# Two layers of experts with Strassen-like products on one core: the order of one sum on VectorE, and two products' tokens split by GpSimd

## The chip, the cores and the metric
The kernel runs on one core of a Trainium2 chip. The metric is the device time of one execution in microseconds; the time of a version is the median of its runs. The profile is of one further execution.

## What is computed
Attention with 4 sink keys and a window of 128, then a mixture of four experts with given weights, then a gated layer `h * cos(h)`. All values are fp32.

```python
x = attention(q, k, v)                  # 2 x 768 tokens, 8 heads of 64: x is 1536 x 512
p = domain_probs / (domain_probs.sum(-1, keepdims=True) + 1e-09)
for e in range(4):                      # w1[e]: 512 x 1024, w2[e]: 1024 x 512
    out += p[:, e:e + 1] * (np.maximum(x @ w1[e], 0.0) @ w2[e])
h = out @ w_in                          # 512 x 2048
result = (h * np.cos(h)) @ w_out        # 2048 x 512
```

## The kernel before
**Precision.** Each fp32 operand is split into a high part (rounded to the type fp32r) and a low part (operand minus high part, also fp32r). A product is then three matmuls: high by high, low by high, high by low (L1278, L1280, L1282 in the first layers; L1306, L1308, L1310 in the second). Making a split is a cast and a subtraction.

**Stages.** After the attention (to about 100 us) the work runs in 24 stages in four blocks. A block is one half of the tokens (768) in one layer pair: stages 0 to 7 and 8 to 15 are the experts for the first and the second half of the tokens, stages 16 to 19 and 20 to 23 the gated layers for the same halves. `FIRST = (0, 8, 16, 20)` holds the first stage of each. A stage takes 512 columns of the first weight and 512 rows of the second, and has two halves, a = 2s and b = 2s + 1.

**First layer of a half.** It is done with seven products of half matrices in place of eight (numbers 1 to 7; 6 matmuls of 128x384 each). The inputs of some are sums of blocks of x (`t_sum`) and of w1 (`w1_sum`), made by GpSimd. The products accumulate along a chain of PSUM banks: 1, then 6, 5 and 3 on top of it in `chain_bank`; 2 in `two_bank`; 7 and then 4 in `side_bank`. Between two of the chain ScalarE copies the bank out: `keep_1` (L694, after product 1), `keep_2` (L701, after 6), `keep_3` (L708, after 5). VectorE makes the four quarters of the result: `add_11` (L994), `add_22` (L1002, from product 7 and `keep_3`), `add_21` (L1010). Product 4 is written on top of `side_bank`, which `add_22` reads, so it waits for `add_22` of its half (L1271).

**Then** each quarter goes through the relu and is split: in an expert stage `relu_hi` on ScalarE (L725), `relu_lo` on VectorE (L1014). In a gated stage it is `whole` (L733), `fraction` (L1022), `fold` (L739), `cosine` (L744), `gate` (L1029), `gated_hi` (L752), `gated_lo` (L1035). `down` (L1306 to L1310, 36 matmuls for each half, 6 for each of six token tiles) is the second layer. VectorE adds the result of each of the six tiles to `acc` with `keep_down` (L1044 to L1050).

**Queues.** Each engine executes its instructions in the order in which they stand in the program; that order is written out by hand. TensorE in a stage: products a1, a2, a6, a7, a5, b1, a3, a4, b6, b2, b5, b7, b3, b4, then `down` of half a and of half b. Names in the rows: `scores` are PSUM banks 0 to 3, `bank` the banks 4 to 7, so product 4 of half b writes a `bank` and product 3 of half b a `scores`. The weights are split in each stage: `first_hi` on ScalarE (L669) and `first_lo` on GpSimd (L555) for w1, in three parts for each half; `second_hi` (L679) and `second_lo` (L562) for w2. GpSimd makes the sums of the next stage's w1 (`sum_weights`, L541 to L550) ahead of its `first_lo`.

**Opening of a block.** At the end of a block (`closes(s)`) the tokens of the next are split for all seven products: `tokens_hi` on ScalarE (L687), `tokens_lo` on VectorE (L952), in the order of `PRODUCTS = (1, 2, 6, 7, 5, 3, 4)`; each is 128x768 elements. At the end of stage 19, VectorE runs products 1 and 2's `tokens_lo`, then alternates the six `keep_down` with the other five, and then begins stage 20 with `add_11(a)`. ScalarE's stage 20 begins with `keep_1(a)`, then `whole` (which waits for `add_11(a)`), then `keep_2(a)`, on which product 5 of half a waits.

Of the kernel before, what the change touches and what calls it, by code (L numbers as in the profile page):

```python
# [5 lines left out]
ALU = mybir.AluOpType  # L6
ACT = mybir.ActivationFunctionType
AX_X = mybir.AxisListType.X
F32 = mybir.dt.float32
# [21 lines left out]
PRODUCTS = (1, 2, 6, 7, 5, 3, 4)  # L31


def program(nc, q, k, v, domain_probs, w1, w2, w_in, w_out, out, routing):
# [8 lines left out]
    TPB = S // P  # L43
# [20 lines left out]
    FIRST = (0, NE, 2 * NE, 2 * NE + NM)  # L64
    NS = 2 * NE + 2 * NM
    DOWN_ORDER = (3, 4, 5, 0, 1, 2)
    TURN_AT = {0: FIRST[1], 1: FIRST[2]}
    SUM_AT = {FIRST[1] - 2: 1, FIRST[2] - 2: 2, FIRST[3] - 1: 3}
    GATED = ((0, 11), (0, 22), (0, 12), (0, 21), (1, 22), (1, 12), (1, 11), (1, 21))

    def block_of(s):
        return sum(s >= first for first in FIRST) - 1
# [26 lines left out]
    with ExitStack() as ctx:  # L99
# [3 lines left out]
        def sem(name):  # L103
            return ctx.enter_context(nc.semaphore(name))

        x_hi = sb("x_hi", [P, 7, 2, HALF], F32R)
# [111 lines left out]
        x_summed = sem("x_summed")  # L218
        x_hi_ready = sem("x_hi_ready")
        x_lo_ready = sem("x_lo_ready")  # L220
        product_done = {n: sem(f"product{n}_done") for n in PRODUCTS}
        kept1 = sem("kept1")
        kept2 = sem("kept2")
# [58 lines left out]
        def x_block(block, n):  # L282

            g = block % 2
            low, high = slice(0, HALF), slice(HALF, S)
            if n in (1, 2):
                return x_t[:, g, 2 * (n - 1):2 * n, low]
            if n == 3:
                return x_t[:, g, 2:4, high]
            if n == 5:  # L290
                return x_t[:, g, 0:2, high]
            return t_sum[:, {6: 0, 7: 1, 4: 2}[n]]

        def w1_part(half, part):

# [132 lines left out]
        def _(pool):  # L428
# [102 lines left out]
            def sum_weights(s, n):  # L531

                low, high = slice(0, FS // 2), slice(FS // 2, FS)
                a11, a12 = w1_raw[:, 0:2, low], w1_raw[:, 2:4, low]
                a21, a22 = w1_raw[:, 0:2, high], w1_raw[:, 2:4, high]
                s2, s3, s4 = (w1_sum[:, i] for i in range(3))
                if n == 0:
                    pool.wait_ge(w1_landed, 16 * (s + 1))
                    if s >= 1:
                        pool.wait_ge(w1_lo_ready, 6 * s)  # L540
                    nc.gpsimd.tensor_tensor(s3, a11, a21, ALU.subtract).then_inc(w1_summed, 1)  # L541
                elif n == 1:
                    pool.wait_ge(w1_summed, 4 * s + 1)
                    nc.gpsimd.tensor_tensor(a21, a21, a22, ALU.add).then_inc(w1_summed, 1)
                elif n == 2:
                    pool.wait_ge(w1_summed, 4 * s + 2)
                    nc.gpsimd.tensor_tensor(s2, a21, a11, ALU.subtract).then_inc(w1_summed, 1)
                else:
                    pool.wait_ge(w1_summed, 4 * s + 3)
                    nc.gpsimd.tensor_tensor(s4, a12, s2, ALU.subtract).then_inc(w1_summed, 1)  # L550
# [14 lines left out]
            def sum_tokens(b, n):  # L565
# [20 lines left out]
                else:  # L586
                    pool.wait_ge(x_summed, 4 * b + 3)
                    nc.gpsimd.tensor_tensor(t4, b21, t2, ALU.subtract).then_inc(x_summed, 1)

            for i in range(ROUNDS + 3):  # L590
                if i % 2 == 0 and 0 <= (i - 2) // 2 < T and later((i - 2) // 2):
                    gather_sinks((i - 2) // 2)
                if 0 <= i - TURN_LAG < ND:
                    part_weights(i - TURN_LAG)
                if i == 0:
                    sink_keys(0)
                    sink_keys(1)
                    spread_values(0)
                elif i % 2 == 1 and (i + 3) // 2 < T:
                    sink_keys((i + 3) // 2)  # L600
                if i in (3, 2 * TPB + 2):
                    lower_values(i // TPB // 2)
                if i == 9:
                    spread_values(1)
                if 5 <= i < 9:
                    sum_weights(0, i - 5)
                if 10 <= i < 16:
                    first_lo(*divmod(i - 10, 3))
                if i % 2 == 0 and 0 <= (i - 6) // 2 < T:
                    normalise((i - 6) // 2)  # L610
                if 17 <= i < 21:
                    sum_tokens(0, i - 17)

            for s in range(NS):
                second_lo(s, 0)
                second_lo(s, 1)
                if s in SUM_AT:
                    for n in range(4):
                        sum_tokens(SUM_AT[s], n)
                if s + 1 < NS:  # L620
                    for n in range(4):
                        sum_weights(s + 1, n)
                    for h in (2 * s + 2, 2 * s + 3):
                        for part in range(3):
                            first_lo(h, part)

        @block.scalar
        def _(act):
# [52 lines left out]
            def tokens_hi(b, i):  # L681

                n = PRODUCTS[i]
                act.wait_ge(x_summed, 4 * (b + 1))
                if b >= 1:
                    act.wait_ge(product_done[n], 2 * FIRST[b])
                nc.scalar.activation(x_hi[:, n - 1], x_block(b, n), ACT.Copy).then_inc(x_hi_ready, 1)  # L687
# [184 lines left out]
        def _(dve):  # L872
# [75 lines left out]

            def tokens_lo(b, i):
                n = PRODUCTS[i]  # L950
                dve.wait_ge(x_hi_ready, 7 * b + i + 1)
                nc.vector.tensor_tensor(x_lo[:, n - 1], x_block(b, n), x_hi[:, n - 1].bitcast(F32), ALU.subtract)\  # L952
                    .then_inc(x_lo_ready, 1)

# [34 lines left out]
            def add_11(h):  # L989

                dve.wait_ge(product_done[2], h + 1)
                dve.wait_ge(kept1, h + 1)
                c = two_bank[h % 2][:, 0:HALF]
                nc.vector.tensor_tensor(c, c, kept[:, h % 2], ALU.add).then_inc(c11_ready, 1)  # L994
# [67 lines left out]
            for s in range(NS):  # L1062
                a, b = 2 * s, 2 * s + 1
                n = 8 * (s - FIRST[2])
                add_11(a)
                if is_gated(s):
                    fraction(n)
                    gate(n)
                    add_22(a)
                    gated_lo(n)  # L1070
                    fraction(n + 1)
                    fraction(n + 2)
                    add_21(a)
                    add_11(b)
                    gate(n + 1)
                    gate(n + 2)
                    fraction(n + 3)
                    add_22(b)
                    gated_lo(n + 1)
                    gated_lo(n + 2)  # L1080
                    fraction(n + 4)
                    gate(n + 3)
                    fraction(n + 5)
                    add_21(b)
                    gated_lo(n + 3)
                    gate(n + 4)
                    fraction(n + 6)
                    gated_lo(n + 4)
                    gate(n + 5)
                    fraction(n + 7)  # L1090
                    gated_lo(n + 5)
                    gate(n + 6)
                    gate(n + 7)
                    gated_lo(n + 6)
                    gated_lo(n + 7)
                else:
                    relu_lo(a, 11)
                    add_22(a)
                    relu_lo(a, 22)
                    relu_lo(a, 12)  # L1100
                    add_21(a)
                    relu_lo(a, 21)
                    add_11(b)
                    relu_lo(b, 11)
                    add_22(b)
                    relu_lo(b, 22)
                    relu_lo(b, 12)
                    add_21(b)
                    relu_lo(b, 21)
                if closes(s):  # L1110
                    for i in range(2 if is_gated(s) else 5):
                        tokens_lo(block_of(s) + 1, i)
                for k in range(TPB):
                    keep_down(s, k)
                    if closes(s) and is_gated(s) and k < 5:
                        tokens_lo(block_of(s) + 1, k + 2)
                    elif closes(s) and k < 2:
                        tokens_lo(block_of(s) + 1, k + 5)
                for i in range(len(turned_tiles(s))):
                    keep_turned(s, i)  # L1120

        @block.tensor
        def _(pe):
# [118 lines left out]
            def product(h, n):  # L1242

                s, i = divmod(h, 2)
                if opens(s) and i == 0:
                    pe.wait_ge(x_lo_ready, 7 * block_of(s) + PRODUCTS.index(n) + 1)
                pe.wait_ge(w1_lo_ready, 3 * h + (1 if n in (1, 2) else 2 if n in (7, 6, 3) else 3))
                if n == 1:
                    target, first = chain_bank[i], True
# [166 lines left out]
```

## Time and profile before
| | us |
|---|---|
| median of the runs | 863.89 |
| lowest and highest of the runs | 863.51, 864.95 |
| the profiled execution, its own time | 860.06 |
| its span, first to last instruction | 858.3 |
| TensorE matmul busy | 842.5 (98% of the span) |
| VectorE busy | 461.1 (54%) |
| ScalarE busy | 458.7 (53%) |
| GpSimd busy | 541.1 (63%) |
| mean granted clock of TensorE | 0.996 |

The engines' names in rows are PE (TensorE matmul), PEld (its weight loads), DVE (VectorE), ACT (ScalarE), POOL (GpSimd), SP (SyncE). A row of the timeline has the start in us from the span's start, the duration in us, engine, line, operation, output and inputs, shapes, the number of instructions merged into it, and in brackets the idle time before it with what ended it. Matmuls are pipelined: the durations of neighbours overlap, so the step from one start to the next is what one costs.

### The profile page before, as it was taken

The page shows a single profiled execution, that of the slowest core. Times are in us where ns is not written, and L with a number is a line of the kernel's source. Part 1 is how long each engine was busy: PE and PEld are TensorE (multiplying, and loading weights), DVE is VectorE, ACT ScalarE, POOL GpSimd, SP SyncE. Part 2 cuts the span into 40 slices and gives each one's busy share as a digit, 9 for nine tenths or more (in the row PEclk, how much of TensorE's full clock was granted, in tenths as well). Part 3 has the DMA queues.
Part 4 walks back from the last instruction along what each step waited for, and adds up shares of the span by engine and source line. Part 5 has one row for each costly group of instructions (what it writes and reads, how often), then busy time and mean ns, then how long its engine had stood idle before and what let it go on. Part 6 is the DMA issues. An engine that isn't in the chain of part 4 may idle for free.

```text
span 858.3 us, 13943 instructions
## 1 busy us (share of the span) xinstructions
PE 842.5 (98%) x4756; PEld 751.0 (87%) x4756; DVE 461.1 (54%) x952; ACT 458.7 (53%) x984; POOL 541.1 (63%) x408
## 2 busy tenths in 40 slices
PE   8899899999999999999999999999999999899998
PEld 6788789989988988988988998998898998898997
DVE  6678633433433427533433433348757759747756
ACT  6587734334334336423423423526867869767864
POOL 3699776556466775675475475867385396584450
PEclk9999999999999999999999999999999999999999
DMA  9794331211311220321131121120220230530201
GB/s 168 175 204 114 98 99 50 99 50 50 99 52 48 98 72 27 99 99 35 65 99 39 60 99 50 50 99 26 73 99 19 81 99 1 173 99 3 96 0 74
DMA packets 73156, 67.31 MB, mean 78 GB/s; under 512 B 40608, under 2 KB 46848, under 8 KB 73088
## 3 DMA queue, kind: packets, MB, share of 16 engines
q1 hardware_dynamic: 73088, 66.42, 26.0%
q8 instruction: 40, 0.66, 0.3%
q14 instruction: 28, 0.23, 0.1%
HBM read 62.96 MB, written 3.19 MB: 77 GB/s over the span
## 4 chain that ended last, share of the span: by engine, by line
PE 90%; issue 3%; DVE 2%; POOL 1%; ACT 1%; DMA 1%; SPq 1%; ACTq 0%; POOLq 0%
PE scores L1278 11%; PE scores L1282 10%; PE scores L1280 10%; PE scores L1308 10%; PE scores L1310 10%; PE scores L1306 10%; PE bank L1308 5%; PE bank L1310 5%; PE bank L1306 5%; PE bank L1278 3%; PE bank L1282 3%; PE bank L1280 3%; PE bank L1224 2%; PE scores L1187 1%; DVE x_lo L952 1%
## 5 line engine op out<-in xcount | busy, mean ns | idle before, releaser
L555 POOL TENSOR_TENSOR w_lo<-w_raw,w_hi 128x512 fp32r<-128x512 f32 x96 | 128.6, 1349 | 184.3 <-ACT w_hi L669 184.3
L1278 PE MATMUL scores<-x_hi,w_hi 128*128 128x384 f32 x528 | 178.6, 338 | 4.0 <-ACT kept L701 2.6
L1282 PE MATMUL scores<-x_hi,w_lo 128*128 128x384 f32 x528 | 177.3, 336 | 0.0
L1280 PE MATMUL scores<-x_lo,w_hi 128*128 128x384 f32 x528 | 177.3, 336 | 0.0
L562 POOL TENSOR_TENSOR w_lo<-w_raw,w_hi 128x1024 fp32r<-128x1024 f32 x48 | 116.8, 2444 | 65.6 <-ACT w_hi L679 65.6
L679 ACT ACTIVATE w_hi<-w_raw 128x1024 fp32r<-128x1024 f32 x48 | 50.7, 1059 | 189.7 <-PE scores L1310 189.7
L1308 PE MATMUL scores<-w_lo,h_hi 128*128 128x512 f32 x384 | 149.7, 390 | 0.0
L1310 PE MATMUL scores<-w_hi,h_lo 128*128 128x512 f32 x384 | 149.7, 390 | 0.0
L1306 PE MATMUL scores<-w_hi,h_hi 128*128 128x512 f32 x384 | 149.4, 389 | 0.0
L1278 PEld LDWEIGHTS scores<-x_hi,w_hi 128*128 128x128 f32 x528 | 99.6, 189 | 6.4 <-issue 5.6
L1050 DVE SCALAR_TENSOR_TENSOR acc<-scores,probs,acc 128x512 f32<-128x512 f32 x56 | 41.8, 749 | 116.3 <-PE scores L1310 116.3
L1280 PEld LDWEIGHTS scores<-x_lo,w_hi 128*128 128x128 f32 x528 | 99.7, 189 | 0.6
L1282 PEld LDWEIGHTS scores<-x_hi,w_lo 128*128 128x128 f32 x528 | 99.7, 189 | 0.0
L555 POOL TENSOR_TENSOR w_lo<-w_sum,w_hi 128x768 fp32r<-128x768 f32 x48 | 92.5, 1927 | 3.1 <-ACT w_hi L669 3.1
L1310 PEld LDWEIGHTS scores<-w_hi,h_lo 128*128 128x128 f32 x384 | 72.1, 188 | 15.0
L1306 PEld LDWEIGHTS scores<-w_hi,h_hi 128*128 128x128 f32 x384 | 72.1, 188 | 14.2
L1308 PEld LDWEIGHTS scores<-w_lo,h_hi 128*128 128x128 f32 x384 | 72.1, 188 | 14.2
L1308 PE MATMUL bank<-w_lo,h_hi 128*128 128x512 f32 x192 | 74.8, 390 | 0.0
L1310 PE MATMUL bank<-w_hi,h_lo 128*128 128x512 f32 x192 | 74.8, 389 | 0.0
L1306 PE MATMUL bank<-w_hi,h_hi 128*128 128x512 f32 x192 | 74.7, 389 | 0.0
L1014 DVE SCALAR_TENSOR_TENSOR h_lo<-bank,h_hi 128x384 fp32r<-128x384 f32 x64 | 35.7, 558 | 47.0 <-ACT h_hi L725 47.0
L1014 DVE SCALAR_TENSOR_TENSOR h_lo<-scores,h_hi 128x384 fp32r<-128x384 f32 x64 | 35.5, 555 | 47.3 <-ACT h_hi L725 45.8
(126 smaller groups left out, 1582.4 us busy)
## 6 DMA issues: line engine op xcount, KB each, us to landing
w_raw<-in_moe_w_dram SPq DMA_DIRECT2D x32, 1024.0 KB, 5.1
w_raw<-in_moe_w_in_dram SPq DMA_DIRECT2D x8, 1024.0 KB, 5.0
w_raw<-in_moe_w_out_dram SPq DMA_DIRECT2D x8, 1024.0 KB, 5.1
v_nat<-in_v_dram SPq DMA_DIRECT2D x12, 256.0 KB, 3.5
norm<-routing_dram SPq DMA_DIRECT2D x24, 128.0 KB, 3.2
out_dram<-acc SPq DMA_DIRECT2D x12, 256.0 KB, 4.2
k_nat<-in_k_dram SPq DMA_DIRECT2D x11, 256.0 KB, 4.8
q_nat<-in_q_dram SPq DMA_DIRECT2D x11, 256.0 KB, 5.2
```

Source lines behind the costliest of these rows:

```text
L555: nc.gpsimd.tensor_tensor(w1_slots(w1_lo, h % 2, part), w1_part(h % 2, part), w1_slots(w1_hi, h % 2, part).bitcast(F32), ALU.subtract)\
L562: nc.gpsimd.tensor_tensor(w2_lo[:, i::2], w2_raw[:, i::2], w2_hi[:, i::2].bitcast(F32), ALU.subtract)\
L679: nc.scalar.activation(w2_hi[:, i::2], w2_raw[:, i::2], ACT.Copy).then_inc(w2_hi_ready, 1)
L1014: nc.vector.scalar_tensor_tensor(h_part(h_lo, h % 2, c), c_source(h % 2, c), 0.0, h_part(h_hi, h % 2, c).bitcast(F32), ALU.max, ALU.subtract)\
L1050: kept_one = nc.vector.scalar_tensor_tensor(acc[:, n], down_bank[k][:], probs[:, n, e:e + 1], acc[:, n], ALU.mult, ALU.add)
L1224: last = nc.tensor.matmul(out_bank[r * D:(r + 1) * D, cols], v_nat[:, (t - 1 + part) % 3, head:head + D], weights_t[:, d % SLOTS, part, 2 ...
L1278: nc.tensor.matmul(target[:, 0:HALF], w1_hi[:, i, slot, d], x_hi[:, n - 1, d], start=first and d == 0, stop=False, skip_group_check=True)
L1280: nc.tensor.matmul(target[:, 0:HALF], w1_hi[:, i, slot, d], x_lo[:, n - 1, d], start=False, stop=False, skip_group_check=True)
L1282: last = nc.tensor.matmul(target[:, 0:HALF], w1_lo[:, i, slot, d], x_hi[:, n - 1, d], start=False, stop=d == 1, skip_group_check=True)
L1306: nc.tensor.matmul(down_bank[k][:], h_hi[:, i, f, toks], w2_hi[:, c], start=i == 0 and f == 0, stop=False, skip_group_check=True)
L1308: nc.tensor.matmul(down_bank[k][:], h_hi[:, i, f, toks], w2_lo[:, c], start=False, stop=False, skip_group_check=True)
L1310: last = nc.tensor.matmul(down_bank[k][:], h_lo[:, i, f, toks], w2_hi[:, c], start=False, stop=i == 1 and f == 1, skip_group_check=True)
```

## The change
1. **Expert stages, VectorE.** In half b, `add_22(b)` now stands ahead of `relu_lo(b, 11)` in place of behind it. The gated stages' order is not touched.
2. **Last block, GpSimd.** The splits of the tokens of products 1 and 2 of block 3 (the one that opens with stage 20) are made by GpSimd, cast and subtraction both, with semaphores of their own. They stand in its queue behind stage 20's `sum_weights` and ahead of its `first_lo`. ScalarE and VectorE leave them out, and the counts on which VectorE and TensorE wait are adapted.

```diff
+    SPLIT_BY_POOL = (1, 2)
...
+        def by_pool(block, n):
+            return block == 3 and n in SPLIT_BY_POOL
+
+        def splits_before(block, i):
+            return 7 * block + sum(not by_pool(block, n) for n in PRODUCTS[:i])
...
+            def split_tokens(b):
+                for m, n in enumerate(SPLIT_BY_POOL):
+                    pool.wait_ge(x2_ready, TPB * (b - 1))
+                    pool.wait_ge(product_done[n], 2 * FIRST[b])
+                    nc.gpsimd.tensor_copy(x_hi[:, n - 1], x_block(b, n)).then_inc(x_hi_ready_pool, 1)
+                    pool.wait_ge(x_hi_ready_pool, m + 1)
+                    nc.gpsimd.tensor_tensor(x_lo[:, n - 1], x_block(b, n), x_hi[:, n - 1].bitcast(F32), ALU.subtract)\
+                        .then_inc(x_lo_ready_pool, 1)
...
                     for n in range(4):
                         sum_weights(s + 1, n)
+                    if s + 1 == FIRST[3]:
+                        split_tokens(3)
                     for h in (2 * s + 2, 2 * s + 3):
...
             def tokens_hi(b, i):
                 n = PRODUCTS[i]
+                if by_pool(b, n):
+                    return
...
             def tokens_lo(b, i):
                 n = PRODUCTS[i]
-                dve.wait_ge(x_hi_ready, 7 * b + i + 1)
+                if by_pool(b, n):
+                    return
+                dve.wait_ge(x_hi_ready, splits_before(b, i) + 1)
...
                     add_11(b)
+                    add_22(b)
                     relu_lo(b, 11)
-                    add_22(b)
                     relu_lo(b, 22)
...
                 if opens(s) and i == 0:
-                    pe.wait_ge(x_lo_ready, 7 * block_of(s) + PRODUCTS.index(n) + 1)
+                    if by_pool(block_of(s), n):
+                        pe.wait_ge(x_lo_ready_pool, SPLIT_BY_POOL.index(n) + 1)
+                    else:
+                        pe.wait_ge(x_lo_ready, splits_before(block_of(s), PRODUCTS.index(n)) + 1)
```

## Rows read from the trace of the kernel before

**Rows 1.** The page, busy times: share of the span and instructions.
```profile
PE 842.5 (98%) x4756; PEld 751.0 (87%) x4756; DVE 461.1 (54%) x952; ACT 458.7 (53%) x984; POOL 541.1 (63%) x408
```

**Rows 2.** Waits of the weight loads: us in total, times, longest.
```profile
PEld bank L1278 <- issue: 5.2, 16, 0.3
```

**Rows 3.** Timeline of TensorE, stage 1: ends of products 7 and 3, start of 4.
```profile
139.87 0.33 PE L1282 MATMUL bank<-x_hi,w_lo 128*128 128x384 f32 x1
...
140.91 0.34 PE L1282 MATMUL scores<-x_hi,w_lo 128*128 128x384 f32 x1
141.29 0.41 PE L1278 MATMUL bank<-x_hi,w_hi 128*128 128x384 f32 x1
141.54 0.34 PE L1280 MATMUL bank<-x_lo,w_hi 128*128 128x384 f32 x1
```

**Rows 4.** Timeline of TensorE at the opening of stage 20.
```profile
730.61 0.34 PE L1282 MATMUL scores<-x_hi,w_lo 128*128 128x384 f32 x1
733.60 0.41 PE L1278 MATMUL scores<-x_hi,w_hi 128*128 128x384 f32 x1 [2.65 <-ACT kept L701]
```

**Rows 5.** Windows: length, busy PE, PEld, DVE, ACT, POOL, granted clock, DMA, GB/s.
```profile
86.20:89.60 3.40, 1.97 (x22) 1.47 (x22) 3.23 (x13) 3.40 (x13) 2.72 (x5) 1.00 0.27 68
...
734.70:738.10 3.40, 3.40 (x13) 3.40 (x12) 1.98 (x4) 2.03 (x5) 3.10 (x3) 0.51 0.33 67
```

**Rows 6.** Timeline of ScalarE, VectorE and weight loads at the same place.
```profile
139.20 0.49 ACT L708 ACTIVATE kept<-scores 128x384 f32<-128x384 f32 x1 [1.21 <-PE scores L1282]
...
140.11 0.56 DVE L1014 SCALAR_TENSOR_TENSOR h_lo<-bank,h_hi 128x384 fp32r<-128x384 f32 x1 [1.05 <-ACT h_hi L725]
140.58 0.56 DVE L1002 TENSOR_TENSOR bank<-bank,kept 128x384 f32<-128x384 f32 x1
...
141.26 0.19 PEld L1278 LDWEIGHTS bank<-x_hi,w_hi 128*128 128x128 f32 x1 [0.33 <-issue]
```

**Rows 7.** Timeline, gated stage 19: end of product 7, the sum, product 4.
```profile
707.98 0.33 PE L1282 MATMUL bank<-x_hi,w_lo 128*128 128x384 f32 x1
...
708.35 0.57 DVE L1002 TENSOR_TENSOR bank<-bank,kept 128x384 f32<-128x384 f32 x1
...
709.19 0.34 PE L1278 MATMUL bank<-x_hi,w_hi 128*128 128x384 f32 x1
```

**Rows 8.** Timeline of ScalarE, VectorE and TensorE, end of stage 19.
```profile
717.70 1.58 ACT L687 ACTIVATE x_hi<-x_t 128x768 fp32r<-128x768 f32 x2
...
718.58 1.91 DVE L952 TENSOR_TENSOR x_lo<-x_t,x_hi 128x768 fp32r<-128x768 f32 x2 [0.17 <-ACT x_hi L687]
...
719.57 0.39 PE L1310 MATMUL scores<-w_hi,h_lo 128*128 128x512 f32 x1
...
720.41 0.68 DVE L1046 TENSOR_TENSOR acc<-scores,acc 128x512 f32<-128x512 f32 x1
...
727.50 2.00 DVE L952 TENSOR_TENSOR x_lo<-x_t,x_hi 128x768 fp32r<-128x768 f32 x1
729.43 0.68 DVE L1046 TENSOR_TENSOR acc<-bank,acc 128x512 f32<-128x512 f32 x1
730.03 1.45 DVE L952 TENSOR_TENSOR x_lo<-t_sum,x_hi 128x768 fp32r<-128x768 f32 x1
...
732.00 0.55 DVE L994 TENSOR_TENSOR scores<-scores,kept 128x384 f32<-128x384 f32 x1
```

**Rows 9.** Timeline of GpSimd, end of stage 19.
```profile
717.51 1.29 POOL L555 TENSOR_TENSOR w_lo<-w_raw,w_hi 128x512 fp32r<-128x512 f32 x1 [5.50 <-ACT w_hi L669]
...
728.64 2.02 POOL L555 TENSOR_TENSOR w_lo<-w_raw,w_hi 128x512 fp32r<-128x512 f32 x1
```

**Rows 10.** Groups of GpSimd by shape: busy us, mean ns of one, idle before.
```profile
L480 POOL TENSOR_SCALAR_AFFINE_SELECT weights_t<-weights_t 128x512 f32<-128x512 f32 x20 | 13.5, 673 | 0.0
...
L585 POOL TENSOR_TENSOR t_sum<-x_t 128x768 f32<-128x768 f32 x4 | 7.4, 1845 | 0.2
...
L491 POOL CAST sink_w<-weights 128x64 fp32r<-128x64 f32 x10 | 3.1, 308 | 0.0
```

More of the change, by code:

```diff
@@ L220, in program @@
         x_lo_ready = sem("x_lo_ready")
+        x_hi_ready_pool = sem("x_hi_ready_pool")
+        x_lo_ready_pool = sem("x_lo_ready_pool")
         product_done = {n: sem(f"product{n}_done") for n in PRODUCTS}
```

## The prediction, made before the change was run
> **What bounds the kernel now.** I read the page's busy times first, then the waits, then the timeline engine by engine. The page gives TensorE 842.5 us of a span of 858.3 us [rows 1]. So the time is TensorE's own, plus the places where it stands still; a change on another engine counts only through such a place. The matmuls of the first layers (L1278, L1280, L1282) start 0.173 us apart when nothing holds them, those of the second (L1306 to L1310) 0.227 us. I went through all starts after 103 us and looked for larger steps. Three kinds matter here.
>
> First, one small step in each of the 16 expert stages, always ahead of product 4 of half b; the list of waits has it as 16 idle stretches of the weight load for `bank` that sum to 5.2 us [rows 2]. In one stage the start at 140.91 should be followed at 141.08 and 141.26; the profile has 141.29 and 141.54 [rows 3]. The second shows what is really lost, 0.285 us: 16 x 0.285 = 4.55 us.
>
> Second, one large stand at the opening of stage 20, the last block: last start 730.61, next 733.60 instead of 730.78, 2.82 us lost [rows 4].
>
> Third, behind this stand the granted clock is about half (0.51, the 1.2 GHz level) for 3.4 us [rows 5]; against 2.4 GHz that costs 3.4 x 0.49 = 1.65 us.
>
> **Part 1, the order on VectorE in an expert stage.** Nothing is added or removed: `add_22(b)` and `relu_lo(b, 11)` change places, 16 times. Before, ScalarE's copy of product 5 ends at 139.69 and TensorE's product 7 at 139.87 + 0.33 = 140.20 [rows 3, 6]. That is all `add_22(b)` needs, but `relu_lo(b, 11)`, started at 140.11, stands ahead of it in the queue, so it starts at 140.58 and ends at 141.14; the weight load follows 0.12 us later, at 141.26 [rows 6]. In the new order it starts 0.04 us behind product 7, at 140.24, ends at 140.80, and the load can go at 140.92. On time would be 140.91: the matmul comes on its beat. The gated stages already have that order, and show it: product 7 ends at 707.98 + 0.33 = 708.31, `add_22` starts at 708.35 and takes 0.57, and product 4 starts at 709.19, on the beat of 0.173 [rows 7]. So the whole step goes: **-4.55 us**. What it costs: `relu_lo(b, 11)` (0.56 us) ends some 0.6 us later, near 141.3. Behind it queue `relu_lo(b, 22)` and the rest of half b. ScalarE's `relu_hi(b, 22)` comes 0.34 us earlier than before, since it waits for `add_22`, so `relu_lo(b, 22)` is no later than before. The reader of `relu_lo(b, 11)` is the second half of `down`, 36 matmuls x 0.227 = 8.2 us behind 142.4: cover of over 8 us, and a delay of 0.6 us would cost 0.6 us a stage if that cover were gone. I count zero. Bounds of the part: 0 (product 4 has a second wait that is as late) to -4.8.
>
> **Part 2, the split by GpSimd at the opening of stage 20.** It removes two casts on ScalarE (`tokens_hi`, 1.58 us the pair) and two subtractions on VectorE (1.91 us the pair) [rows 8], and adds a cast and a subtraction on GpSimd for each of products 1 and 2. They stand ahead of `first_lo(40, 0)`. Their waits are long met; nothing but the GpSimd queue is behind them.
> GpSimd's time: it is idle for 5.50 us ahead of 717.51, thus from 712.01 [rows 9]. A subtraction of 128x768 takes 1.85 us [rows 10]. A cast of that size isn't in the trace. Rows near it: 673 ns for a pass over 512 columns with one input, 308 ns for a cast of 64 columns in short pieces [rows 10]. Taking 0.2 us as fixed part, the first scales to 0.91 us, the second to 1.5; the second taken as it stands, 12 x 0.308, gives 3.7 at worst, and no cast can beat the first much. I take 1.0, near the first, as this read has no short pieces. Then 2 x (1.0 + 1.85) = 5.7: done at 717.7, where `first_lo(40, 0)` could start at 717.51. A delay of 0.2 us.
> The Trainium skill, "GPSIMD Engine Reference", section "4.1 Engine selection", says that elementwise work on two inputs belongs on VectorE, as GpSimd is about 2x slower. The trace agrees on the price, 1.85 against 0.95; by that rule alone the move loses 1.8 us, and here it doesn't, as the queue stood idle. The same table calls one-input work roughly line rate, which would be 0.8 us for the cast, an estimate of that page.
> What opens the stand is VectorE. TensorE's product 5 waits for `keep_2(a)` on ScalarE, that queues behind `whole`, that waits for `add_11(a)`, that is queued behind six `keep_down` (0.60 us each to the next) and five `tokens_lo`. `keep_down` from 729.43 to 730.03 shows the 0.60 us. From `add_11` at 732.00 to product 5 at 733.60 it is 1.60 us [rows 4, 8]. The two removed subtractions lie at the front, but the first `keep_down` can't start before its bank is done, 719.57 + 0.39 + 0.04 = 720.00 [rows 8]; it started at 720.41. So of 1.91 us only 0.41 lies on the path.
> The rest hangs on how the two engines share the memory. A `tokens_lo` with GpSimd mostly idle takes 0.95 us (the pair at 718.58) [rows 8], beside GpSimd 1.45 or 2.00. The rows fit one reading: it waits until GpSimd's running instruction ends, then needs 0.78 us, and GpSimd's next one stands for that time. GpSimd's change at 728.64 gives 729.42, the row started at 727.50 is followed at 729.43 [rows 8, 9]; all five rows fit so. With that I laid out the new stretch (0.60 for a `keep_down`, for GpSimd's subtractions of 512 and 768 columns 1.25 and 1.82 us, which are 1.29 and 1.85 less the overlap of two in a row [rows 9, 10]): GpSimd 717.70 to 718.95 to 720.77; `tokens_lo` done at 721.55; GpSimd 722.77, next done 723.55; 724.77, 725.55; 727.34, 728.12; 729.34, 730.12; last `keep_down` 730.12 to 730.72, and product 5 at 730.72 + 1.60 = 732.32. Gain 1.28 us, **-1.3**. It moves with the cast: at 0.9 us between -0.8 and -1.4 (the first `tokens_lo` may fall behind one more GpSimd instruction), at 1.8 us a loss of 0.3, at 3.7 us a loss of 1.05. Bounds: -1.4 to +1.05.
> The stand would shrink from 2.65 us (730.95 to 733.60) to 1.4. Elsewhere, in 86.20 to 89.60, TensorE stood still for 3.40 - 1.97 = 1.43 us and the clock stayed at 1.00 [rows 5]. So the half clock behind it probably goes too: **-1.65**. Bounds 0 and -1.65.
> The semaphore waits added on TensorE (products 1 and 2 of stage 20) are met by 717.7, needed from 726.60 on. SyncE's load of the next first weights waits for `first_lo`, which ends about 1 us earlier than before: no loss.
>
> **Sum.** -4.55 - 1.3 - 1.65 = -7.5 us, on an execution of 860.06 us (span 858.3): 852.6. The median of the timed runs is 863.89, 3.8 us above; I know no row for this difference and carry the change over as it is: 863.89 - 7.5 = **856.4 us**.
>
> **Rivals.**
> 1. The clock still falls behind the shorter stand: -5.85, **858.0 us**. For it: 1.4 us in one piece is not what 86.20 shows, where it was in several.
> 2. GpSimd is late by 1 to 2 us and meets VectorE wrongly: part 2 gives nothing or loses up to 1.05, the clock falls as before: **859.3 to 860.4**.
> 3. Part 1 doesn't do what it says, because something as late as `add_22` holds product 4 (w1's low part, product 7 itself). Only part 2 stays: **861 us**, or no change with rival 2. Against it: the gated stages' rows.
> 4. Slower: the cast on GpSimd is far dearer than its neighbours. Product 1 of stage 20 needs `first_lo(40, 0)` behind both splits, so TensorE stands at 726.60 once the splits end after 725.3, and from there each us of a cast costs two. Splits end at 712.01 + 3.7 + 2c; the loss eats part 1's 4.55 us and 1.7 more at about c = 9 us, and c = 12 us would give about **871 us**. Against it: the 308 ns row.
>
> **Chances.** Forecast 0.52; rival 1 0.22; rival 2 0.15; rival 3 0.08 (half of it within 0.2%); rival 4 0.03. A measurement of this kernel can tell about 0.2% (1.7 us) from no change. So faster 0.92, same 0.05, slower 0.03. The range is from 855.6 (cast well met, part 1 at its upper bound) to 860.4 (rival 2); it leaves out rivals 3 and 4.
>
> **What would show it.** Right: no step of more than 0.05 us ahead of product 4 in any expert stage, `add_22(b)` starting within 0.1 us of product 7's end, each expert stage shorter by 0.28 us. At stage 20: splits done on GpSimd near 717.7 less the 4.55 us, first `keep_down` 0.04 us behind its bank, product 5 about 1.5 us late and not 2.8, granted clock 1.00 behind it. Wrong: product 4 still held in expert stages by another releaser; a GpSimd cast above 1.5 us; `tokens_lo` durations that don't end 0.78 us behind a GpSimd instruction; half clock still there.

## The result, and the profile after

| | before | after |
|---|---|---|
| median of the runs, us (4 each) | 863.83 | 854.24 |
| lowest and highest | 863.51, 864.95 | 853.72, 856.62 |
| ratio, with its 95% interval | | 0.9892 (0.9871 to 0.9913) |
| profiled execution, us (span) | 860.06 (858.3) | 853.72 (852.0) |

The change gains 9.6 us by the medians. The forecast was 7.5, 856.4 us with a range from 855.6: the sign was right, and the time lies 1.4 us under the range. The two profiled executions differ by 6.3 us only (the one after is also the fastest of its four). So three numbers ask for an explanation, 9.6, 7.5 and 6.3, and what follows is about them. "Stand" is used for a time in which TensorE stands still, "half clock" for a granted clock of 0.5, the 1.2 GHz level. (Rows 6 of before, "at the same place", are at the place of rows 3.)

The busy times of the page:

```profile
PE 838.0 (98%) x4756; PEld 750.9 (88%) x4756; DVE 458.6 (54%) x950; ACT 458.4 (54%) x982; POOL 546.0 (64%) x412
```

VectorE and ScalarE have two instructions less each, GpSimd four more.

**The expert stages.** Timeline of TensorE and VectorE at the place of rows 3 and 6 (lines have moved: 1278 is now 1308, 1280 1310, 1282 1312; `add_22` is L1029, `relu_lo` L1041):

```profile
140.65 0.33 PE L1312 MATMUL bank<-x_hi,w_lo 128*128 128x384 f32 x1
...
141.69 0.34 PE L1312 MATMUL scores<-x_hi,w_lo 128*128 128x384 f32 x1
141.86 0.34 PE L1308 MATMUL bank<-x_hi,w_hi 128*128 128x384 f32 x1
142.04 0.33 PE L1310 MATMUL bank<-x_lo,w_hi 128*128 128x384 f32 x1
...
141.02 0.57 DVE L1029 TENSOR_TENSOR bank<-bank,kept 128x384 f32<-128x384 f32 x1 [1.18 <-PE bank L1312]
141.49 1.21 DVE L1041 SCALAR_TENSOR_TENSOR h_lo<-bank,h_hi 128x384 fp32r<-128x384 f32 x2
```

Product 7 ends at 140.65 + 0.33 = 140.98, the sum starts 0.04 us later, and product 4 follows at 141.86 and 142.04, on the beat of 0.17. The steps of 0.38 and 0.25 us of rows 3 are gone, in this stage and in the 15 others; the list of waits has no `bank` row of L1308 left among its first.

**The opening of stage 20.** GpSimd, VectorE and TensorE (L606 is the new cast, L608 the new subtraction, L979 `tokens_lo`, L1073 `keep_down`, L1021 `add_11`; answers to rows 4, 8 and 9):

```profile
708.69 0.83 POOL L606 CAST x_hi<-x_t 128x768 fp32r<-128x768 f32 x1
709.59 1.86 POOL L608 TENSOR_TENSOR x_lo<-x_t,x_hi 128x768 fp32r<-128x768 f32 x1
...
712.30 1.85 POOL L608 TENSOR_TENSOR x_lo<-x_t,x_hi 128x768 fp32r<-128x768 f32 x1
714.24 1.29 POOL L566 TENSOR_TENSOR w_lo<-w_raw,w_hi 128x512 fp32r<-128x512 f32 x1
715.49 1.85 POOL L566 TENSOR_TENSOR w_lo<-w_sum,w_hi 128x768 fp32r<-128x768 f32 x1
717.34 2.12 POOL L566 TENSOR_TENSOR w_lo<-w_raw,w_hi 128x512 fp32r<-128x512 f32 x1
...
716.73 0.69 DVE L1073 TENSOR_TENSOR acc<-scores,acc 128x512 f32<-128x512 f32 x1 [1.60 <-PE scores L1340]
717.34 0.95 DVE L979 TENSOR_TENSOR x_lo<-t_sum,x_hi 128x768 fp32r<-128x768 f32 x1
...
727.25 0.55 DVE L1021 TENSOR_TENSOR scores<-scores,kept 128x384 f32<-128x384 f32 x1
...
727.35 0.34 PE L1312 MATMUL scores<-x_hi,w_lo 128*128 128x384 f32 x1
728.85 0.41 PE L1308 MATMUL scores<-x_hi,w_hi 128*128 128x384 f32 x1 [1.17 <-ACT kept L726]
```

The cast costs 0.83 us, the first `keep_down` waits for its bank and nothing else, and product 5 is 1.33 us late (727.35 to 728.85 less 0.17) where it was 2.82. The granted clock behind it is full. Behind the stand in the attention part it is half, as it was in before (windows: length, busy PE, PEld, DVE, ACT, POOL, granted clock, DMA, GB/s):

```profile
28.00:33.90 5.90, 2.32 (x28) 1.72 (x28) 2.25 (x12) 2.14 (x9) 3.41 (x6) 1.00 0.96 171
33.90:37.30 3.40, 3.40 (x24) 2.99 (x22) 1.81 (x10) 1.48 (x6) 3.40 (x6) 0.50 0.21 63
728.80:732.20 3.40, 3.35 (x19) 3.38 (x20) 1.85 (x5) 2.96 (x6) 3.28 (x3) 1.00 0.46 175
```

**The balance of the two profiles.** From the first matmul of the second layer (111.18 before, 111.95 after) to the last (854.71, 848.38) the changed kernel is 7.1 us shorter. Set against each other matmul by matmul, the two profiles place all of it: 15 steps of 0.27 us (4.1), 1.5 of the stand, 1.6 of the clock. So an expert step cost 0.27 us, not the 0.285 that the prediction read off printed starts, and 16 of them 4.35. The stretch ahead holds one more step that the change takes away, and yet this stretch is 0.77 us longer. The 1.05 us in between lie in the attention part, which the change doesn't touch. There TensorE waits for `sink_w`, queued on GpSimd behind the first sum of w1, which waits for that weight's load. The two waits in the changed kernel:

```profile
POOL w_sum L552 <- DMA w_raw<-in_moe_w_dram: 6.5, 1, 6.5
...
PE bank L1192 <- POOL sink_w L505: 3.6, 1, 3.6
```

In before the longest wait for `sink_w` was 2.5 us and that for the load 5.4; the 1.1 us between 3.6 and 2.5 are the 1.05 us.

### The profile page after: what moved, and what is told of

Same layout as the page of the kernel before. It is cut to its first block, busy times and chain, and to the rows that moved or that the text cites. A ratio compares the mean times of both kernels' runs of the same rounds, so it can differ in the third digit from the quotient of the medians.

```text
span 852.0 us, 13943 instructions
## 1 busy us (share of the span) xinstructions
PE 838.0 (98%) x4756; PEld 750.9 (88%) x4756; DVE 458.6 (54%) x950; ACT 458.4 (54%) x982; POOL 546.0 (64%) x412
## 4 chain that ended last, share of the span: by engine, by line
PE 94%; issue 2%; DVE 2%; ACT 1%; POOL 1%; DMA 0%; POOLq 0%; ACTq 0%
PE scores L1308 11%; PE scores L1312 10%; PE scores L1310 10%; PE scores L1340 10%; PE scores L1338 10%; PE scores L1336 10%; PE bank L1338 5%; PE bank L1340 5%; PE bank L1336 5%; PE bank L1308 3%; PE bank L1310 3%; PE bank L1312 3%; PE bank L1251 2%; PE scores L1214 2%; PE bank L1227 1%
## 5 line engine op out<-in xcount | busy, mean ns | idle before, releaser
L1308 PE MATMUL scores<-x_hi,w_hi 128*128 128x384 f32 x528 | 177.8, 337 | 2.5 <-ACT kept L726 1.2
L1308 PEld LDWEIGHTS scores<-x_hi,w_hi 128*128 128x128 f32 x528 | 99.1, 188 | 4.9 <-issue 4.1
L1041 DVE SCALAR_TENSOR_TENSOR h_lo<-scores,h_hi 128x384 fp32r<-128x384 f32 x64 | 35.5, 555 | 47.3 <-ACT h_hi L750 45.8
L692 ACT ACTIVATE w_hi<-w_raw 128x512 fp32r<-128x512 f32 x96 | 57.7, 622 | 2.6 <-POOL w_sum L561 2.6
```

The costliest lines, as they stand in the source:

```text
L692: nc.scalar.activation(w1_slots(w1_hi, h % 2, part), w1_part(h % 2, part), ACT.Copy)\
L1041: nc.vector.scalar_tensor_tensor(h_part(h_lo, h % 2, c), c_source(h % 2, c), 0.0, h_part(h_hi, h % 2, c).bitcast(F32), ALU.max, ALU.subtract)\
L1308: nc.tensor.matmul(target[:, 0:HALF], w1_hi[:, i, slot, d], x_hi[:, n - 1, d], start=first and d == 0, stop=False, skip_group_check=True)
```

## The experiments

**1. How far do executions of one kernel differ?** The kernel before, once more, on one chip (which chip the first measurement ran on isn't on record).

> The kernel before, unchanged, to see how one execution differs from the next. The changed kernel gained 9.6 us by the medians but only 6.3 us between the two profiled executions, since the profiled execution of before (860.06) was 3.8 us below its median. Theory A: the timed executions of before differ from the profiled one outside the changed places, in the attention part: there TensorE stood 2.47 us in one profile and 3.58 us in the other for a sum that waits for the first load of w1, and a stretch of half clock followed. Then executions spread by 1 to 4 us, the mean granted clock goes with them (0.996 against 0.998 is one more stretch of 3.4 us at half clock, 1.7 us), and the median of this kernel can be anywhere from 860 to 865. Theory B: the typical execution loses more at the changed places than the profiled one. Then another profile of it shows more than 2.82 us lost at stage 20 or more than 0.285 us in an expert stage.

Ten executions took 859.31 to 866.95 us, 33 of the same kernel beside them on that chip 858.67 to 865.75. The mean granted clock of an execution goes with its time. Of the 33, at 0.998 the mean of 4 was 859.75, at 0.996 that of 12 861.93, at 0.994 that of 11 864.14 us. From one such level to the next the time moves by 2.2 us; 1.7 of them are lost clock (0.002 x 860), one stretch of 3.4 us at half clock. In this profile the stand at stage 20 lost 2.78 us, each expert step 0.27 us: the changed places are as in the first. What differs is ahead of stage 0's second layer, which began at 113.84 instead of 111.18. Theory A holds; B finds nothing in this profile. A median of four, as in the first measurement, is uncertain by more than the 0.2% that the prediction named: drawn again and again from all 74 later executions of this kernel, such medians have a standard deviation of 1.2 us.

**2. The two parts, each alone, and both again,** on that chip.

```diff
                     add_11(b)
+                    add_22(b)
                     relu_lo(b, 11)
-                    add_22(b)
```

> Only the exchange of the sum and the low part in the expert stages, the split of the last block as before. By the rows of the changed kernel all 16 steps of 0.285 us go: 4.6 us, and nothing else; the stand at stage 20 stays at 2.8 us and the half clock behind it mostly too. Ratio about 0.9947. If theory B holds (timed executions lose more at the expert stages), 6 us or more. If the exchange only helps together with the split: under 4.

857.56 us, ratio 0.9946 (0.9925 to 0.9967), 12 executions. The mean was 857.58 against 862.67 of before, 5.1 us less; forecast 4.6. In its profile the expert steps are gone and the stand at stage 20 is there with 2.78 us, this time with full clock behind it.

The second is the changed kernel with the order in the expert stages as before:

```diff
                     add_11(b)
-                    add_22(b)
                     relu_lo(b, 11)
+                    add_22(b)
```

> Only the split of products 1 and 2 by GpSimd, the order in the expert stages as before. The stand at stage 20 goes from 2.82 to 1.33 us, and with it the stretch of half clock behind it: 1.5 + 1.65 = 3.1 us, ratio about 0.9964. If the clock is at half behind the shorter stand in some executions, 1.5 to 3. If the part of the gain that is open (some 2 us) comes from stage 20, 5 us.

860.64 us, ratio 0.9987 (0.9968 to 1.0007): less than forecast, and not clear of nothing. The profile lost 1.98 us at stage 20, not 1.33, and its attention part had two stretches of half clock in a row.

> The changed kernel, unchanged, on the same chip as the two halves. If the parts add up: the sum of both, 7.7 us, ratio 0.991; the ratio of 0.9892 that was measured first would then hold about 2 us that belong to no part of the change. If they help each other: 9.6 us again with halves that sum to less.

855.66 us, ratio 0.9929 (0.9904 to 0.9954). By means 6.2 us, near the sum of the parts (5.1 + 1.4 = 6.5): they add. The 9.6 us of the first measurement didn't come again. Its profile shows the second value of the stand, 1.98 us, and why:

```profile
716.65 1.29 POOL L566 TENSOR_TENSOR w_lo<-w_raw,w_hi 128x512 fp32r<-128x512 f32 x1
717.91 1.85 POOL L566 TENSOR_TENSOR w_lo<-w_sum,w_hi 128x768 fp32r<-128x768 f32 x1
719.75 1.30 POOL L566 TENSOR_TENSOR w_lo<-w_raw,w_hi 128x512 fp32r<-128x512 f32 x1
...
719.77 2.08 DVE L979 TENSOR_TENSOR x_lo<-t_sum,x_hi 128x768 fp32r<-128x768 f32 x1
721.78 0.68 DVE L1073 TENSOR_TENSOR acc<-bank,acc 128x512 f32<-128x512 f32 x1
722.38 0.94 DVE L979 TENSOR_TENSOR x_lo<-t_sum,x_hi 128x768 fp32r<-128x768 f32 x1
```

In the first profile VectorE's subtraction and GpSimd's third started in the same moment, 717.34; VectorE's took 0.95 us, GpSimd's 2.12. Here GpSimd is 0.02 us ahead: 1.30 us for it, 2.08 for VectorE. The loser waits for the whole instruction of the winner. The recorded starts tell the winner only roughly: in the last kernel of experiment 6 GpSimd's row starts at 714.59 and VectorE's at 714.60, and VectorE had the first turn (0.95 us against 2.11). The prediction had named this as the edge of its layout ("may fall behind one more GpSimd instruction").

**3. Do the engines take turns by whole instructions?** Two versions of the changed kernel with more casts on GpSimd ahead of the second product's subtraction, executed once each (859.65 and 860.99 us), for their profiles alone. The first:

```diff
+        extra_casts = sem("extra_casts")
...
                     pool.wait_ge(x_hi_ready_pool, m + 1)
+                    if m == 1:
+                        nc.gpsimd.tensor_copy(x_hi[:, n - 1], x_block(b, n)).then_inc(extra_casts, 1)
+                        pool.wait_ge(extra_casts, 1)
+                        nc.gpsimd.tensor_copy(x_hi[:, n - 1, 0, 0:384], x_block(b, n)[:, 0, 0:384]).then_inc(extra_casts, 1)
+                        pool.wait_ge(extra_casts, 2)
```

> The changed kernel with two more casts on GpSimd (768 and 384 columns, about 0.90 and 0.58 us) ahead of the second product's subtraction: GpSimd is 1.5 us later. Theory (a subtraction of VectorE waits until GpSimd's running instruction ends, then takes 0.8 us, and GpSimd's next one stands for that time): laid out by hand, TensorE's stand ahead of product 5 is 2.8 us. Rival (both engines are slowed in proportion while they overlap): VectorE's five subtractions take the same sum of 7.3 us as in the changed kernel, the stand is 1.3 to 1.5 us. Rival (GpSimd's delay is passed on): 1.33 + 1.5 = 2.8 as well; the next run tells these apart.

The stand cost 2.49 us, VectorE's five subtractions took 2.10, 1.45, 1.44, 2.00 and 1.45. The second has 768, 768 and 128 columns in place of 768 and 384:

> As the run before, with three more casts (768, 768 and 128 columns, together 2.2 us). By the theory of taking turns a longer delay costs less here, as VectorE's first subtraction now falls into the end of GpSimd's first, short instruction instead of the start of its second, long one: stand 2.25 us, and the first subtraction of VectorE takes 1.2 to 1.3 us. If the delay is passed on: 3.5 us. In proportion: 1.3 to 1.5.

The stand cost 1.96 us, less than with the shorter delay:

```profile
722.39 1.02 DVE L987 TENSOR_TENSOR x_lo<-t_sum,x_hi 128x768 fp32r<-128x768 f32 x1
...
723.93 2.01 DVE L987 TENSOR_TENSOR x_lo<-t_sum,x_hi 128x768 fp32r<-128x768 f32 x1
```

Both are 0.3 us under the number laid out, and the first subtraction took 1.02 us where 1.2 to 1.3 was expected. But the order of the two is that of the theory, and neither rival has it: a delay passed on would give 3.5 in the second, a slowing in proportion about 1.4 in both. Turns by whole instructions hold. The second version had half clock behind its stand of 1.79 us; no shorter one at this place had.

**4. Can the rest of the stand go?** The last split behind `add_11(a)` of stage 20:

```diff
                 add_11(a)
+                if s == FIRST[3]:
+                    tokens_lo(3, 6)
...
-                    if closes(s) and is_gated(s) and k < 5:
+                    if closes(s) and is_gated(s) and k < 4:
                         tokens_lo(block_of(s) + 1, k + 2)
```

> The changed kernel, and the last split on VectorE (tokens_lo of product 4 of the last block) behind add_11(a) of stage 20 instead of ahead of the last keep_down. It takes 1.4 us out of the queue ahead of add_11; product 4 of half a comes 7 us later and doesn't wait for it. If the VectorE queue is what holds product 5, the stand of 1.33 or 1.98 us goes to 0 or 0.6, and no half clock stands behind it: 1.4 to 2.5 us faster than the changed kernel. If the stand is ScalarE's or GpSimd's: no change.

855.84 us, ratio 0.9941 (0.9916 to 0.9965), on another chip: of the 1.4 to 2.5 us expected over the changed kernel nothing can be seen (its ratios were 0.9929 and 0.9892 in its two measurements). The stand ahead of product 5 did go down to 0.59 us, as expected, but 1.63 us came up ahead of product 3. VectorE:

```profile
725.75 0.55 DVE L1021 TENSOR_TENSOR scores<-scores,kept 128x384 f32<-128x384 f32 x1
726.21 2.73 DVE L979 TENSOR_TENSOR x_lo<-t_sum,x_hi 128x768 fp32r<-128x768 f32 x1
728.86 0.55 DVE L1049 SCALAR_TENSOR_TENSOR angles<-scores,angles 128x384 f32<-128x384 f32 x1
```

The moved split meets GpSimd's longest instruction (`second_lo`, 1024 columns) and takes 2.73 us; `fraction` queues behind it, ScalarE's `fold` and `cosine` wait for that, `keep_3` (L733) queues behind them, and product 3 waits for `keep_3`. A wait took the place of the one removed.

**5. The attention part.** The sums of the first w1 and what follows them, two rounds later, in the changed kernel:

```diff
-                if 5 <= i < 9:
-                    sum_weights(0, i - 5)
-                if 10 <= i < 16:
-                    first_lo(*divmod(i - 10, 3))
+                if 7 <= i < 11:
+                    sum_weights(0, i - 7)
+                if 12 <= i < 18:
+                    first_lo(*divmod(i - 12, 3))
...
-                if 9 <= i < 15:
-                    first_hi(*divmod(i - 9, 3))
+                if 11 <= i < 17:
+                    first_hi(*divmod(i - 11, 3))
```

> The changed kernel, and in the attention part the four sums of the first w1 (sum_weights(0), queued on GpSimd from round 5) and the casts and low parts behind them two rounds later. So GpSimd no longer stands for the first load of w1 with the sink columns queued behind it, for which TensorE stood 2.5 to 5 us in all profiles so far, each time with one or two stretches of half clock. If the open 2 us of the first measurement are the chance of that place (each execution has one to four stretches of half clock, 1.7 us each, and the time goes with them), the stand at 28 to 33 us and the half clock behind it are gone: 3.5 to 6 us faster than the changed kernel, all executions at a granted clock of 0.998 or more, and a much smaller spread than the 5 us of before. If the chance sits elsewhere: spread and clock as before, gain under 2 us.

852.38 us, ratio 0.9891 (0.9868 to 0.9914), beside experiment 4 on the same chip. The granted clock was 0.998 or more in five of the six executions and 0.997 in the slowest, of 856.08 us, and the second layer of stage 0 began at 109.14. Against before that is 9.3 us where the changed kernel had 6.9 on its chip: some 2.5 us more, less than the 3.5 to 6 expected. The stand at stage 20 was 1.99 us here.

**6. The whole change without that chance.** Four kernels of one set, on another chip, all with the edit of experiment 5: without the change, with its first part, with its second, with both (the kernel of experiment 5 again).

> The kernel before with only the sums of the first w1 two rounds later on GpSimd, nothing of the change. With the four kernels of this set, which all have it, the parts of the change can be weighed without the chance of the attention part. By theory A the executions agree within 2 us and come 3 us under before, near 859; the half clock behind the stand of 2.65 us at stage 20 is left as the one chance.

> As the first of this set, with the exchange in the expert stages. 16 steps of 0.285 us less: 4.6 us under the first. If 5 or more, the exchange does something besides that step.

> As the first of this set, with the split by GpSimd. The stand at stage 20 is 1.33 or 1.98 us instead of 2.82, by which engine takes the turn at the same moment: 0.8 to 1.5 us, and up to 1.65 more in the share of executions in which half clock stood behind it. Mean 1.0 to 2.5 under the first. Rival: the open 2 us of the first measurement belong here; then 3.5 or more.

> The changed kernel with the sums two rounds later, again. If the parts only add: 5.5 to 7 us under the first of this set, near 852.5. If they help each other, more than the sum of the two before it.

| | median, us | lowest to highest | mean clock | lost at stage 20 in the profile |
|---|---|---|---|---|
| without the change (12) | 858.85 | 857.34 to 859.64 | 0.997 to 1.0 | 2.81, half clock behind |
| order (6) | 854.17 | 853.40 to 854.78 | 0.997 to 1.0 | 2.81, full clock |
| split (6) | 855.83 | 855.17 to 856.63 | 0.999 to 1.0 | 1.33, full clock |
| both (6) | 851.05 | 850.32 to 852.33 | 0.999 to 1.0 | 1.33, full clock |
| the kernel before beside them (17) | 863.18 | 859.60 to 867.80 | 0.992 to 0.998 | |

The executions of a kernel now agree within 2.3 us, not 8. By medians the order gains 4.7 us (forecast 4.55), the split 3.0 (forecast 1.3 and 1.65), both 7.8 (forecast 7.5); by means 4.7, 2.9 and 7.4. The parts add. The expectations written for the split (1.0 to 2.5) and for both (5.5 to 7) were lower than what came; they had allowed for the longer of the two stands and for less from the clock. The record shows what the clock gave: without the split, 13 of the 18 executions of this set had a mean clock of 0.998 or less, with it none of 12. The means of the clock, 0.9983 without the change and 0.9997 with the split, differ by 1.1 us of 860; with the 1.5 us of the shorter stand that is 2.6 of the 2.9 us. The last is the fastest version of this study, ratio 0.9861 (0.9831 to 0.9890) against before, 12 us. Windows of its profile, over the same stretches as those of the changed kernel above:

```profile
28.00:33.90 5.90, 5.90 (x73) 4.97 (x73) 5.21 (x25) 4.37 (x19) 2.76 (x5) 1.00 1.08 194
33.90:37.30 3.40, 3.40 (x46) 2.88 (x46) 2.79 (x13) 2.59 (x10) 3.32 (x6) 1.00 0.97 222
```

5.90 us busy of 5.90, where it was 2.32, and 46 matmuls in the next 3.4 us instead of 24.

## Why the prediction was right in its steps and wrong in its number

**Part 1: right.** The step in each expert stage (0.27 us), `add_22` 0.04 us behind product 7, product 4 on its beat, nothing behind the later `relu_lo`: all as worked out. By the profiles it gives 4.35 us, by the times 5.1 where executions scatter and 4.7 where they scatter little, against 4.55. Reading the answer off the gated stages [rows 7], which had the new order already, was what made this term safe; rival 3 is out.

**Part 2, the cast: right, on the cheap side.** 0.83 us instead of 1.0 [rows 10]. The Trainium skill, "GPSIMD Engine Reference", section "4.1 Engine selection", calls one-input work roughly line rate; the estimate of 0.8 us by it was nearer than the one from rows. Rivals 2 (as a late GpSimd) and 4 are out.

**Part 2, VectorE's queue: right in mechanism, and between two values.** Of the two subtractions' 1.91 us only a part came back, since the first `keep_down` waits for its bank. Turns by whole instructions stood the test of experiment 3. The forecast of 1.28 us came from a cast of 1.0. With 0.83 the layout has a tie in it, and a tie of 0.02 us decides between 1.5 and 0.8 us; the first lies just outside the part's bound of 1.4. Of the six profiles with the split and no other edit at this place, three lost 1.33 us and three 1.98 or 1.99: too few for a share.

**The clock behind the stand: right in sign, and a chance.** With the stand of 2.65 us half clock came with it in three of five profiles; with the split in one of nine, the one with the longer delay. By the clocks of experiment 6 the share is much the same, 13 of 18 against none of 12; in experiment 5, with a stand of 1.99 us in its profile, two of six executions were at 0.998 or less, where in them isn't on record. So rival 1 was mostly wrong, but isn't out. 1.65 us is what the half clock costs when it comes. That the one profile of before had it was luck: over executions the term is nearer 1.1 us.

**The number: the failed step is the last one of the sum,** "I know no row for this difference and carry the change over as it is". The 3.8 us between the profiled execution and the median were the row to look for. It was there: the chain of waits begins with a long wait of GpSimd for the first load of w1, TensorE stood 2.5 us behind it, and the granted clock fell to half. The prediction began its search at 103 us, where the change starts, and so never read the part that scatters most. The later executions of before took 856.9 to 867.8 us, at a mean clock of 1.0 to 0.992; those of the changed kernel 853.7 to 859.6. The first measurement had four of each. Those of the changed kernel had clocks of 0.998, 0.998, 0.998 and 0.996; those of before, 863.5 to 865.0 us, sat where later executions with 0.994 sit, but their own clocks are not known, so this last link is argued, not shown. Medians of four drawn from the 74 later executions of before and the 8 of the changed kernel differ by 6.5 us in the mean, with a standard deviation of 1.7, and by 9.6 or more in 1.5 of 100 draws; around the 7.8 of experiment 6 it would be one draw in seven. So scatter can make 9.6 of 7.8, but that it alone did so stays open. What is shown: the same change measured 9.6, 6.9 (by medians; 6.2 by means) and 7.8 us in three measurements, and the last, with the chance taken out, is 0.3 us from the forecast by medians and 0.1 by means. The range had no term for the scatter of medians of four; two of the standard deviations above, 3.4 us on either side, would have been its size. Its lower end was not worked out either: the parts at their bounds (4.8, 1.4 and 1.65) give 856.0, not 855.6.

## What to carry to other kernels

A wait that a sister stage doesn't have is worth a look at that stage's order: the cure and its proof stand in the same profile. Moving an elementwise instruction to an idle GpSimd frees the other queue only up to the next thing that queue waits for, and where both engines then work on SBUF with two inputs, lay the turns out one by one; their sum is not monotonic in a delay. Before carrying a sum over to a median, compare the profiled execution with it, and if they differ by more than the change is worth, find the place that scatters first, even if the change doesn't touch it.

## What the runs showed of the hardware

VectorE's and GpSimd's subtractions with two inputs in SBUF exclude one another for whole instructions. VectorE's of 128x768 took 0.95 us alone, 1.45 or 2.0 us in turns, and 2.73 us behind a long one; GpSimd's of 128x512 took 2.02 to 2.12 us in place of 1.29 where it had to wait. The Trainium skill, "GPSIMD Engine Reference", section "1. Specifications", names the shared interfaces and the case of two SBUF inputs; the runs agree, by the numbers just given. GpSimd's casts, with one input, ran at 0.83 us beside VectorE instructions that read PSUM, and neither was slowed.

TensorE's clock fell from its 2.4 to its 1.2 GHz level for 3.4 us with stands, but not with each: at stage 20 with stands of 2.65, 2.61, 2.65 and 1.79 us, not with 2.61, 2.64, 2.32, 1.82, 1.81, 1.81, 1.46 and three of 1.17 or 1.16. In three of the four the fall came 0.6 to 1.3 us after TensorE had gone on, in the other (experiment 6, without the change) 0.6 us before. In the attention part one to three such stretches, some of them in a row (6.8 us), came after the stand for w1's load in nine profiles of nine; the two of experiment 3 had a second stand for `sink_w` there, of 1.85 and 2.62 us, at which the later ones began. None came in the five profiles without the stand for w1's load. With it gone, executions of one kernel differed by 2.3 us in experiment 6 where those of before, beside them, differed by 8.2; their clocks, 0.992 to 0.998, make 5 us of that.
